# Expert vectors normalised in the fill of an attention, mixture-of-experts and feed-forward kernel, and an earlier comparison of logits

## The reference

```
f = 1 / (1 + exp(-f_logit))
state = f[t] * state + outer(k[t], v[t]);   y[t] = q[t] @ state      # every step t
x  = y with the heads side by side                                    # [3072, 384]
xn = x / (norm(x) + 1e-6);   en = expert_emb / (norm(expert_emb) + 1e-6)
logits = xn @ en.T / tau
expert = argmax(logits);   gate = softmax(logits)[expert]
x  = gate * (relu(x @ w1[expert]) @ w2[expert])                       # w1 384x1024, w2 1024x384
out = ((x @ w_a) * (x @ w_b)) @ w_out                                 # w_a, w_b 384x1536
```

## Time and profile before

| | us |
|---|---|
| median of 3 runs | 829.28 (828.17 to 830.2) |
| the profiled execution, its own time | 828.33 |
| its span | 826.6 |
| PE busy | 805.7 (97% of the span) |
| PE weight loads busy | 731.4 (88%) |
| DVE busy | 362.8 (44%) |
| ACT busy | 323.6 (39%) |
| POOL busy | 140.1 (17%) |
| PE's share of the chain that ended last | 96% |
| DMA | 67.60 MB, mean 82 GB/s |

### The profile page before, as it was taken

One profiled execution on the slowest core, in us unless ns is written; L12 is line 12 of the kernel. 1 busy time (PEld: TensorE's weight loads), 2 busy tenths in 40 slices (PEclk: granted clock), 3 DMA queues, 4 the chain that ended last, 5 costly groups with the idle time before them and its releaser, 6 DMA issues.

```text
span 826.6 us, 14410 instructions
## 1 busy us (share of the span) xinstructions
PE 805.7 (97%) x5348; PEld 731.4 (88%) x5349; DVE 362.8 (44%) x590; ACT 323.6 (39%) x616; POOL 140.1 (17%) x206
## 2 busy tenths in 40 slices
PE   5999998799999999999999999999999999999998
PEld 4999987799999999997888888888888888888887
DVE  6788887855544545355532322232222223222221
ACT  5677766544534445455522322222222212212211
POOL 4444440414232413000000100010010001001001
PEclk9999999799999999999999999999999999999999
DMA  9877762565562555220000100010010001000001
GB/s 204 194 207 199 193 189 71 126 218 203 199 206 88 189 195 184 84 77 2 1 1 1 39 0 1 1 39 0 1 39 1 1 0 39 1 1 15 24 1 39
DMA packets 32574, 67.60 MB, mean 82 GB/s; under 512 B 12145, under 2 KB 21390, under 8 KB 31374
## 3 DMA queue, kind: packets, MB, share of 16 engines
q1 hardware_dynamic: 28174, 55.93, 22.5%
q0 software_dynamic: 4352, 11.04, 4.2%
HBM read 57.48 MB, written 9.48 MB: 81 GB/s over the span
## 4 chain that ended last, share of the span: by engine, by line
PE 96%; DVE 1%; DMA 1%; issue 1%; ACT 0%; POOL 0%; DVEq 0%
PE low_banks L1056 18%; PE scores L1056 18%; PE sums L1063 9%; PE high_banks L1063 9%; PE sums L998 9%; PE low_banks L987 6%; PE scores L987 6%; PE high_banks L998 4%; PE scores L823 3%; PE sums L839 3%; PE high_banks L812 2%; PE low_banks L798 2%; PE sums L830 2%; PE low_banks L806 1%; PE high_banks L850 1%; PE low_banks L967 1%
## 5 line engine op out<-in xcount | busy, mean ns | idle before, releaser
L574 POOL DMA_INDIRECT out<-out_sb,placed x24 | 23.3, 970 | 470.5 <-ACT out_sb L769 464.7
L1056 PE MATMUL low_banks<-x_hi,wab_hi 128*128 128x512 f32 x216 | 84.1, 389 | 1.0 <-issue 1.0
L1056 PE MATMUL low_banks<-x_hi,wab_lo 128*128 128x512 f32 x216 | 84.7, 392 | 0.0
L1056 PE MATMUL scores<-x_hi,wab_lo 128*128 128x512 f32 x216 | 84.7, 392 | 0.0
L1056 PE MATMUL scores<-yT_lo,wab_hi 128*128 128x512 f32 x216 | 84.6, 392 | 0.0
L1056 PE MATMUL low_banks<-yT_lo,wab_hi 128*128 128x512 f32 x216 | 84.6, 392 | 0.0
L1056 PE MATMUL scores<-x_hi,wab_hi 128*128 128x512 f32 x216 | 84.0, 389 | 0.0
L1450 DVE TENSOR_TENSOR h<-low_banks,a_sb 128x512 f32<-128x512 f32 x36 | 24.9, 692 | 133.9 <-ACT a_sb L752 133.9
L1450 DVE TENSOR_TENSOR h<-scores,a_sb 128x512 f32<-128x512 f32 x36 | 24.9, 692 | 130.4 <-ACT a_sb L752 118.0
L752 ACT ACTIVATE a_sb<-low_banks 128x512 f32<-128x512 f32 x36 | 21.5, 597 | 139.3 <-PE low_banks L1056 139.3
L752 ACT ACTIVATE a_sb<-scores 128x512 f32<-128x512 f32 x36 | 21.5, 597 | 134.7 <-PE scores L1056 134.7
(11 more groups left out here) (233 smaller groups left out, 1856.3 us busy)
## 6 DMA issues: line engine op xcount, KB each, us to landing
w_raw<-in_w SPq DMA_DIRECT2D x8, 1536.0 KB
w_raw<-in_w SPq DMA_DIRECT2D x32, 384.0 KB
tok<-in_tok SPq DMA_DIRECT2D x48, 192.0 KB, 3.2
qk_all<-in_chan SPq DMA_DIRECT2D x48, 192.0 KB, 3.4
xd<-xst SPq DMA_DIRECT2D x24, 192.0 KB, 1.9
wab_raw<-in_wab SPq DMA_DIRECT2D x6, 768.0 KB, 6.6
wout_raw<-in_wout SPq DMA_DIRECT2D x1, 1536.0 KB, 6.7
wout_raw<-in_wout SPq DMA_DIRECT2D x1, 768.0 KB, 4.3
```

Of the source, the lines that this page charges most:

```text
L574: pool.indirect_dma_start(out=out, out_offset=bass.IndirectOffsetOnAxis(ap=placed[:, u * B + t, 0:1].bitcast(i32), axis=0), in_=out_sb[:, ...
L1056: last_op = pe.matmul(bank[2 * i + m][:, :], w[:, KM * m + k, cols], moving, start=(k == 0 and w is wab_hi and x is not None), stop=(k == ...
```

## The change

The norms and the division of the expert vectors move from the end of the attention into iteration b = 3 of the fill. The root is made as exp(0.5 ln s), with functions of the table that is loaded already, and corrected on DVE by one Newton step, (s/r + r)/2 + 1e-6. ACT scales the vectors from `emb3` into `emb2`, and PE transposes `emb2` after the outputs and state sums of the iteration, no longer before them. The logits then need no factor: `best_first` loses its multiplication. Diagonal, spreading matmul, PSUM copy and reciprocal at the end are gone. For the first 20 tiles `best_first` stands in `last_chunk` between the logits of tile 20 and the mask of tile 22, and `best_second` after `steep`, ahead of the branch. The start of a block is kept in float16 and without the offset of 1.

```diff
-    block_start = sb("block_start", [P, TILES])
+    block_start = sb("block_start", [P, TILES], f16)
...
+    r["start"] = sb("r_start", [P, TILES], f16)
+    r["blocks"] = sb("r_blocks", [P, TILES])
...
@@ ACT, chunk(), at the head of an iteration @@
+                if first and b == 3:
+                    act.wait_ge(emb_squared, 1)
+                    act.activation(r["embn"][0:E, 1:2], r["embn"][0:E, 0:1], ACT.Ln).then_inc(emb_norm, 1)
+                    act.wait_ge(emb_norm, 1)
+                    act.activation(r["embn"][0:E, 2:3], r["embn"][0:E, 1:2], ACT.Exp, scale=0.5).then_inc(emb_rooted, 1)
                 if not last:
                     act.wait_ge(f_loaded[b], c * 16 + 16)
                     act.activation(e_neg[i][:, :], tok[b][:, 1, :], ACT.Exp, scale=-1.0,
...
                     act.activation(grow[i][:, :, :], grow[i][:, :, :], ACT.Exp).then_inc(grow_ready, 1)
+                if first and b == 3:
+                    act.wait_ge(emb_steps, 4)
+                    act.activation(r["emb2"][0:E, :], r["emb3"][0:E, :, :, :].rearrange("p a h d -> p (a h d)"), ACT.Copy,
+                                   scale=r["embn"][0:E, 5:6]).then_inc(emb_scaled, 1)
...
                     if last and b == 0:
-                        act.wait_ge(emb_squared, 1)
-                        act.activation(r["embn"][0:E, 1:2], r["embn"][0:E, 0:1], ACT.Sqrt).then_inc(emb_norm, 1)
-                        act.wait_ge(emb_norm, 1)
-                        act.activation(r["diag"][0:E, :], ident[0:E, 0:E], ACT.Copy, scale=r["embn"][0:E, 1:2], bias=1e-6 / E).then_inc(norms_ready, 1)
...
-                            if m == TILES - 2:
-                                act.wait_ge(norms_spread, 1)
-                                act.activation(r["norm8"][:, :], bank[7][:, 448:448 + E], ACT.Copy).then_inc(norms_kept, 1)
@@ PE, chunk() @@
-                if first and b == 3:
-                    pe.wait_ge(emb_loaded, 80)
-                    for a in range(HP):
-                        last_op = pe.transpose(bank[7][:, E * a:E * a + E], r["emb3"][0:E, a, :, :].rearrange("p h d -> p (h d)"), ident[0:E, 0:E])
-                    last_op.then_inc(embT_done, 1)
                 if not (first and b < 3):
                     from_state((b - 3) % B)
                     from_scores(m - 3, (b - 3) % B, c + (b == B - 1))
                     state_sums(m - 3, (b - 3) % B, early=first)
+                if first and b == 3:
+                    pe.wait_ge(emb_scaled, 1)
+                    for a in range(HP):
+                        last_op = pe.transpose(bank[7][:, E * a:E * a + E], r["emb2"][0:E, P * a:P * a + P], ident[0:E, 0:E])
+                    last_op.then_inc(embT_done, 1)
@@ PE, last_chunk() @@
-            pe.wait_ge(norms_ready, 1)
             pe.wait_ge(x_ready, TILES - 2)
-            pe.matmul(bank[7][:, 448:448 + E], ones[0:E, :], r["diag"][0:E, :], start=True, stop=True).then_inc(norms_spread, 1)
...
-            pe.wait_ge(norms_kept, 1)
@@ DVE, best_first() @@
-            products = r["zn"][:, some, :]
-            then(dve.tensor_tensor(products, r["z"][:, some, :], over(row(r["inv8"][:, :]), three), ALU.mult))
+            products = r["z"][:, some, :]
@@ DVE, chunk() @@
                 if first and b == 3:
+                    square_embeddings()
                     unit_columns()
...
                     keys(m - 1, (b - 1) % B, c + (b > 0))
                 if first and b == 3:
-                    square_embeddings()
+                    root = r["embn"]
+                    dve.wait_ge(emb_rooted, 1)
+                    dve.reciprocal(root[0:E, 3:4], root[0:E, 2:3]).then_inc(emb_steps, 1)
+                    dve.wait_ge(emb_steps, 1)
+                    dve.tensor_scalar(root[0:E, 4:5], root[0:E, 0:1], root[0:E, 3:4], root[0:E, 2:3], ALU.mult, ALU.add).then_inc(emb_steps, 1)
+                    dve.wait_ge(emb_steps, 2)
+                    dve.tensor_scalar(root[0:E, 4:5], root[0:E, 4:5], 0.5, 1e-6, ALU.mult, ALU.add).then_inc(emb_steps, 1)
+                    dve.wait_ge(emb_steps, 3)
+                    dve.reciprocal(root[0:E, 5:6], root[0:E, 4:5]).then_inc(emb_steps, 1)
@@ DVE, last_chunk() and finish_tiles() @@
             logits(TILES - 4, xz)
+            dve.wait_ge(z_kept, EARLY)
+            best_first(0, EARLY, link)
             mask(TILES - 2, 2)
...
             dve.tensor_scalar(steep[:, :], bank[6][:, 511:512], P - 0.5, None, ALU.is_lt).then_inc(steep_ready, 1)
+            dve.wait_ge(const_ready, SETUP)
+            best_second(0, EARLY, link)

         def finish_tiles():
-            dve.wait_ge(const_ready, SETUP)
-            dve.wait_ge(z_kept, EARLY)
-            dve.wait_ge(norms_kept, 1)
-            link(dve.reciprocal(r["inv8"][:, :], r["norm8"][:, :]))
-            best_first(0, EARLY, link)
             logits(TILES - 3, last_xz[1])
             logits(TILES - 2, last_xz[2])
-            best_second(0, EARLY, link)
             logits(TILES - 1, last_xz[3])
@@ DVE, behind the last tile @@
-        link(dve.tensor_tensor(r["start"][:, :], r["slotf"][:, :], r["low"][:, :], ALU.subtract))
+        link(dve.scalar_tensor_tensor(out=r["start"][:, :], in0=r["slotf"][:, :], scalar=-1.0, in1=r["low"][:, :], op0=ALU.add, op1=ALU.subtract))
```

More of the change, by code:

```diff
@@ L185, in attention_moe_ffn @@
                             l=[P, TILES, E], ex=[P, TILES, E], sm=[P, TILES], sm2=[P, TILES],
-                            token=[P, TILES], low=[P, TILES], start=[P, TILES]).items():
+                            token=[P, TILES], low=[P, TILES]).items():
         r[name] = sb("r_" + name, shape)
     off = sb("off", [P, TILES - BY_DVE, P], f16)
+    r["start"] = sb("r_start", [P, TILES], f16)
+    r["blocks"] = sb("r_blocks", [P, TILES])
     r["pre"] = sb("r_pre", [P, 1 + E * TILES], f16)
@@ L192, in attention_moe_ffn @@
     kT = [sb(f"kT{b}", [P, HP, P]) for b in range(B)]
-    for name, shape in dict(emb2=[P, HP * P], embn=[P, 4], emb3=[P, HP, 2, 64], diag=[P, E], norm8=[P, E], inv8=[P, E]).items():
+    for name, shape in dict(emb2=[P, HP * P], embn=[P, 6], emb3=[P, HP, 2, 64]).items():
         r[name] = sb("r_" + name, shape)
@@ L236, in attention_moe_ffn @@
     embT_done = sem("embT_done")
-    emb_squared, emb_ready, norms_ready, norms_spread, norms_kept = map(
-        sem, ("emb_squared", "emb_ready", "norms_ready", "norms_spread", "norms_kept"))
+    emb_squared, emb_rooted, emb_steps, emb_scaled, emb_ready = map(
+        sem, ("emb_squared", "emb_rooted", "emb_steps", "emb_scaled", "emb_ready"))
     zero_written = sem("zero_written")
@@ L1112, in square_embeddings @@
             flat = r["emb3"][0:E, :, :, :].rearrange("p a h d -> p (a h d)")
-            dve.tensor_tensor_reduce(r["emb2"][0:E, :], flat, flat, 1.0, 0.0, ALU.mult, ALU.add, r["embn"][0:E, 0:1]).then_inc(emb_squared, 1)
+            dve.tensor_tensor_reduce(r["emb2"][0:E, :], flat, flat, 1.0, 1e-30, ALU.mult, ALU.add, r["embn"][0:E, 0:1]).then_inc(emb_squared, 1)
         dve.wait_ge(const_ready, FOR_DVE)
@@ L1423, in _ @@
         dve.tensor_scalar(pairs[:, :, 0].bitcast(i32), row_no[:, :], float(MIDDLE - 1), None, ALU.add)
-        link(dve.tensor_scalar(r["start"][:, :], r["start"][:, :], 1.0 / P, -1.0 / P, ALU.mult, ALU.add))
-        dve.scalar_tensor_tensor(out=place_row[:, :], in0=r["low"][:, :], scalar=float(TILES), in1=r["start"][:, :],
+        link(dve.tensor_scalar(r["blocks"][:, :], r["start"][:, :], 1.0 / P, None, ALU.mult))
+        dve.scalar_tensor_tensor(out=place_row[:, :], in0=r["low"][:, :], scalar=float(TILES), in1=r["blocks"][:, :],
                                  op0=ALU.mult, op1=ALU.add)
```

4 lines of the change are left out of this document (2 added, 2 removed).

## The result

The changed kernel takes 832.97 us (median of 22 runs, 828.21 to 835.53); the kernel before, run beside it, 829.10 (22 runs, 827.67 to 830.50). The ratio is 1.0038, 95% interval 1.0026 to 1.0051: slower by 2.2 to 4.2 us. The forecast was 832.2 and slower. The profiled execution is the fourth longest of the 22 of the changed kernel: 834.15, span 832.8, against 828.33 and 826.6 before. So the two profiles differ by 6.2, more than the medians (3.9), and have to be read for their parts and not for the size.

A forecast was written before the change was run, and what follows sets the result against it. PE was taken to bound nearly every slice, leaving the fill and the serial chain before the first expert matmul. 2.55 + 1.2 - 0.85 = +2.9 on 828.33 gave 831.2, plus 0.95 of scatter 832.2 us; range 829.7 to 834.1.

The forecast's parts named there:

- The stall by ACT's order: Fill: ACT's wait for the late-loaded squares holds queued exponents, delaying PE's transposes by 2.55 us, bounded by 2.2 and 2.9.
- The clock: Fill: PE's rise to 2.4 GHz comes later after the gap, costing 1.2 us; bounds 0.7 and 3.6, or -0.85 if early.
- The end: End of the attention: shorter PE and DVE chains ahead of the gathers and w2 loads gain 0.85 us.
- The clock behind the attention: No term in the sum; the runs' median 0.95 us above the profiled execution was read as scatter of the clock.
- The steps on DVE: End of the attention: DVE gains 0.70 us by spreading the comparison and 0.22 by dropping a multiplication, together 0.92.
- ACT would be next: End of the attention: ACT's `in_low`, moved only 0.31 us to 142.88, end after DVE's at 142.81, leaving 0.85.
- `hit`: DVE operation given float16 operands: taken as 0 gain, with 0.3 us of gain as the other end.
- the forecast's own range: Time if the forecast itself holds: 831.1 to 834.0 us, chance 0.62.
- the rival with the early clock: Fill: the clock rises before PE's gap and outlives it, net +0.85 us, 830.1; chance 0.18.

The follow-up runs named there:

- kernel 3: Changed kernel with ACT's Ln and Exp of the norms moved from the head of the fourth iteration to behind `grow`: 829.36 us, ratio 1.0009 to before.
- kernel 4: Changed kernel with four more 128 x 128 matmuls, results unused, on PE ahead of its wait for the scaled vectors: 829.21 us, ratio 1.0000 to before.
- kernel 2: Kernel before with only the changed fill; old end kept, so logits are divided twice and routing changes: 837.56 us, ratio 1.0111, not comparable in time.
- kernel 9: Kernel before with only the changed fill, its old end working on a diagonal of ones to keep the reference routing: 829.92 us, ratio 1.0023.
- kernel 6: Changed kernel, small loads issued earlier, DVE squaring in its third-iteration wait and making root steps ahead of the unit columns: 828.19 us, ratio 0.9981 to before.
- kernel 5: Changed kernel with the five small loads issued earlier in SP's order, other engines' orders unchanged: 830.49 us, ratio 1.0010 to before.
- kernel 7: Kernel before with 128 x 128 matmuls, results unused, in PE's waits of the fill: 827.73 us, ratio 0.9984.
- 8: Kernel 6 with 128 x 128 matmuls, results unused, in PE's waits of the fill: 827.81 us, ratio 0.9987 to before.

## Why the prediction was right

The direction and the mechanism were right: a stall on PE by ACT's order, and a clock that rises later because of it. That the median came as close as 0.8 us to the forecast is in part luck. In the profiled execution the terms were off by 0.70 too much (the gap), 2.07 too little (the clock), 0.33 too little (the end gave less) and 1.5 that was not in the sum, and its own time, 834.15 against a forecast of 831.2, lies just outside the range; the median is lower because other executions lost less.

- **The stall by ACT's order** was as predicted and shown by kernel 3. Its size was 1.85 instead of 2.55, below my lower bound of 2.2. The load landed at 16.6, 1.25 earlier than in the profile of before; from the start of the square to the transposes it took 6.65 (16.62 to 23.27) instead of the 6.1 that I had summed. So 2.55 - 1.25 + 0.55 = 1.85. The half microsecond that the sum lacked is mainly `kT`: I took 0.68, from a row in which POOL was idle, and it was 1.34 beside POOL's queries.
- **The clock** was the mis-sized term: 1.2 forecast, 3.27 measured, inside the bound of 3.6 that I had from the first rise in the fill, and far from the 3.2 us of delay behind the attention to which I had moved my value. Kernel 4 shows that it is the clock, and that it is caused by the gap. The Trainium skill ("TensorE: Matmul & The Clock Gate", "The HAM clock gate") has idleness bring the slow clock back, with a phase that differs from run to run. The fall in kernel 2 agrees, and so do the 7.3 us that the runs of the changed kernel span.
- **The clock behind the attention** cost 1.5 more in the profiled execution. I had put such differences down as scatter. That is not shown: it is absent in the profiles of before, 2, 4 and 9 and there in all others, nine of them with the new end.
- **The end** was forecast at 0.85, and in the two profiles it gave 0.31 + 0.21 = 0.52. The steps on DVE were right: the 0.39 by which the last `r_z` comes sooner behind PE (0.70 less PE's 0.31) and the 0.22 of the multiplication. That ACT would be next was right too, but I had it 0.07 behind DVE; it was idle 0.23 longer around its branch than before, and was 0.29 behind. At the end of the inversion the gain was 0.31 + 0.37 = 0.68; the term that the sum lacked is the fetching of the rows, which kept 0.16 of it. In the times the gain is not shown at all: kernel 6 is 0.7 to 2.4 us faster, but its fill alone can explain that.
- `hit` took 0.76 with float16 operands, as before: no gain, as assumed.
- The chances: the median lies in the forecast's own range, 831.1 to 834.0. Single executions can follow the rival with the early clock, as kernel 9's profile does. In each profile with ACT's changed order (the changed kernel, 2, 4, 5 and 9) PE waited, 0.94 to 2.52.

## What to carry to other kernels

Ahead of a wait that is put at the head of an engine's iteration, list what stands behind it on that engine, and compare the time at which the wait can end (here a DMA's landing, read from whoever waits for it today) with the time at which that work is wanted. The gap on TensorE during the start of this kernel cost its length and, on top, the delay of the clock's rise, which was the larger part; a few matmuls in the gap, with results that nobody uses, removed the clock's part. What is gained early has to be followed to the next late arrival: kernel 7 began the loop 3.3 us earlier and ended 0.6 earlier. Where runs scatter more after a change than before, look for such a clock in the durations of equal matmuls before looking at the mean.

## What the runs showed that was not expected

- A product of two SBUF operands on DVE (128x512) took 0.68 alone and 1.34 beside POOL's product of 1.27 us; four small copies took 0.85 alone and 1.94 beside it in kernel 3. The one that started first kept its time (kernels 6 and 8, the square and POOL's product). The Trainium skill ("SBUF — State Buffer", "Terms") has the two engines exclude each other on a shared pair of ports; the rows agree.
- The clock fell after a gap of 2.52 (kernel 2) and survived ones of 1.10 (kernel 9) and 1.23 (kernel 4). With a gap of only 0.94 it was late where it had not been up before the gap (kernel 5).
- The same small load landed before 15.8 (kernels 3 and 9), at 16.6 (the changed kernel), at 17.3 (kernel 4) and at 17.85 (before) in different executions with the same order of loads.
- From ACT's last square to its table load, with the branch on `steep` between them, it took 2.70 to 3.05 us.
- The time of this kernel depends on the routing: undivided expert vectors cost 38 us.
